# The first low passes of a group one slot on, layer 2's weight pairs in other slots, and the last two pieces on VectorE

## The reference

```python
X = np.fft.rfft(x, axis=1)                       # along the 3008 tokens
y = np.fft.irfft(X * (filt_r + 1j * filt_i), n=x.shape[1], axis=1)
x = y.reshape(6016, 256)
h = x @ w_in                                     # layer 1: 256 -> 2048
g = np.maximum(h, 0) + alpha * np.minimum(h, 0)
x = g @ w_out                                    # 2048 -> 256
h = np.maximum(x @ w_in2, 0)                     # layer 2
out = h * h @ w_out2
```

## Time and profile before

| | |
|---|---|
| median of three runs | 1165.58 us |
| the profiled execution, its own time | 1166.48 us |
| its span, first to last instruction | 1164.7 us |
| TensorE busy | 1130.4 us, 97% |
| VectorE busy | 971.0 us, 83% |
| ScalarE, GpSimd busy | 654.2 and 606.6 us |
| mean granted TensorE clock | 0.991 |

### The profile page before, as it was taken

The page is one execution under the profiler, slowest core; times in us unless marked ns, Lnnn a source line. Parts: engine busy times, 40 slices in busy tenths (PEclk is TensorE's granted clock), DMA queues, the critical chain, the costliest instruction groups (busy, mean ns, idle before and its releaser), DMA issues.

```text
span 1164.7 us, 17117 instructions
## 1 busy us (share of the span) xinstructions
PE 1130.4 (97%) x6867; PEld 984.8 (85%) x6867; DVE 971.0 (83%) x1116; ACT 654.2 (56%) x769; POOL 606.6 (52%) x440
## 2 busy tenths in 40 slices
PE   7879999999999999999999999999999999999997
PEld 2556888888898898898899899998999989889896
DVE  0769788888878988989888988889888888888886
ACT  4746556565655555555555555555555555555553
POOL 0605544555555665566564554555455455555544
PEclk9989999999999999999999999999999999999999
DMA  8973352544203204313135801101101110110100
GB/s 246 280 232 96 95 142 61 122 119 101 57 28 106 87 21 131 106 44 106 50 107 183 283 3 37 36 1 36 37 7 31 36 36 1 36 37 1 37 18 18
DMA packets 64304, 93.45 MB, mean 80 GB/s; under 512 B 5344, under 2 KB 50272, under 8 KB 64224
## 3 DMA queue, kind: packets, MB, share of 16 engines
q1 hardware_dynamic: 64224, 92.35, 27.4%
HBM read 55.90 MB, written 36.44 MB: 79 GB/s over the span
## 4 chain that ended last, share of the span: by engine, by line
PE 75%; DVE 11%; ACT 4%; issue 4%; DMA 4%; POOL 1%; SPq 0%; POOLq 0%; DVEq 0%; ACTq 0%; PEldq 0%
PE bank L875 13%; PE bank L880 13%; PE bank L876 13%; PE bank L905 12%; PE bank L900 10%; PE bank L898 10%; DVE g_lo L746 4%; PE bank L857 3%; ACT g_hi L503 3%; DVE ct L735 1%; DVE ct L731 1%; DMA v_rows<-v_out_b 1%; DVE ct L740 1%; PE bank L831 1%; PE bank L825 1%
## 5 line engine op out<-in xcount | busy, mean ns | idle before, releaser
L491 POOL TENSOR_TENSOR g_raw<-g_raw 128x250 f32<-128x250 f32 (+1 forms) x192 | 277.1, 1443 | 474.2 <-DVE g_raw L769 474.2
L746 DVE TENSOR_TENSOR g_lo<-g_raw,g_hi 128x1750 fp32r<-128x1750 f32 (+1 forms) x192 | 419.9, 2187 | 38.9 <-ACT g_hi L503 37.6
L594 ACT ACTIVATE g_raw<-bank 128x500 f32<-128x500 f32 (+1 forms) x384 | 226.8, 591 | 378.3 <-PE bank L880 377.1
L503 ACT ACTIVATE g_hi<-g_raw 128x1750 fp32r<-128x1750 f32 (+1 forms) x192 | 320.4, 1669 | 37.8 <-POOL g_raw L494 36.1
L898 PE MATMUL bank<-g_hi,w_hi 128*128 128x250 f32 (+1 forms) x1344 | 321.2, 279 | 1.2 <-ACT g_hi L503 1.2
L900 PE MATMUL bank<-g_hi,w_lo 128*128 128x250 f32 (+1 forms) x1344 | 321.5, 279 | 0.0
L875 PE MATMUL bank<-in_hi,w_hi 128*128 128x500 f32 (+1 forms) x768 | 308.2, 401 | 4.9 <-DVE g_raw L762 4.8
L876 PE MATMUL bank<-in_hi,w_lo 128*128 128x500 f32 (+1 forms) x768 | 298.9, 389 | 0.0
L494 POOL TENSOR_TENSOR g_raw<-g_raw 128x250 f32<-128x250 f32 (+1 forms) x192 | 262.8, 1369 | 15.0
L898 PEld LDWEIGHTS bank<-g_hi,w_hi 128*128 128x128 f32 x1344 | 253.9, 189 | 8.9 <-ACT g_hi L503 1.4
L900 PEld LDWEIGHTS bank<-g_hi,w_lo 128*128 128x128 f32 x1344 | 254.0, 189 | 7.4
(11 more groups left out here) (55 smaller groups left out, 529.1 us busy)
## 6 DMA issues: line engine op xcount, KB each, us to landing
filt_b<-filt SPq DMA_DIRECT2D x36, 256.0 KB, 4.7
vc<-v_rows SPq DMA_DIRECT2D x24, 288.0 KB, 5.0
t_raw_b<-t_rows SPq DMA_DIRECT2D x24, 256.0 KB, 4.5
v_rows<-v_out_b SPq DMA_DIRECT2D x24, 256.0 KB, 3.3
w_rows<-s_hi SPq DMA_DIRECT2D x8, 704.0 KB, 3.8
w_rows<-s_lo SPq DMA_DIRECT2D x8, 704.0 KB, 3.2
w_hi<-w_rows SPq DMA_DIRECT2D x8, 704.0 KB, 4.2
w_lo<-w_rows SPq DMA_DIRECT2D x8, 704.0 KB, 5.7
```

The lines of the kernel that those rows point to most:

```text
L491: pool.tensor_tensor(g_raw[:, r, T2, 0:h], g_raw[:, r, B22, 0:h], g_raw[:, r, T1N, 0:h], ALU.add).then_inc(t2_ready, 1)
L503: return act.activation(dst, src, ACT.Copy)
L594: act.activation(g_raw[:, r, 2 * j:2 * j + 2, 0:h], h_ps[j][:, 0:2 * h].rearrange("p (j d) -> p j d", j=2), ACT.Relu, scale=-1.0 if n < SL ...
L746: dve.tensor_tensor(g_lo[:, q, B11:T4 + 1, 0:h], g_raw[:, q, B11:T4 + 1, 0:h], g_hi[:, q, :, 0:h], ALU.subtract).then_inc(g_lo_ready, 1)
```

## The change

Three things are changed.

1. For n = 8g, g from 1 on, down(n) is cut in two. Its high passes stay in slot n + 2. Its low passes go into slot n + 3, between the two up passes.
2. W2_SLOT, the slots of the eight weight pairs, becomes 37, 43, 50, 58, 66, 74, 82, 90 instead of 40, 46, ... 82. The last store now falls behind layer 1's last slot, so the stores and loads leave the condition on layer 1, and reading back waits for the store of its own pair alone.
3. In the very last slot, VectorE makes the two pieces of L491 and L494, ahead of the g_lo of slot 190.

```diff
-W2_SLOT = [40 + 6 * q for q in range(FP)]
+W2_SLOT = [37, 43, 50, 58, 66, 74, 82, 90]
...
-                    sp.wait_ge(s_stored, 32 * FP)
+                    sp.wait_ge(s_stored, 32 * (q + 1))
...
+                if n == 2 * SLOTS_1 - 1:
+
+                    break
                 pool.wait_ge(t13_ready, n + 1)
                 pool.tensor_tensor(g_raw[:, r, T2, 0:h], g_raw[:, r, B22, 0:h], g_raw[:, r, T1N, 0:h],
...
-            act.wait_ge(t4_ready, 2 * SLOTS_1)
+            act.wait_ge(t4_last, 1)
...
+                if n == 2 * SLOTS_1 - 1:
+                    dve.wait_ge(t13_ready, n + 1)
+                    dve.tensor_tensor(g_raw[:, r, T2, 0:h], g_raw[:, r, B22, 0:h], g_raw[:, r, T1N, 0:h],
+                                      ALU.add).then_inc(t2_last, 1)
+                    dve.wait_ge(t2_last, 1)
+                    dve.tensor_tensor(g_raw[:, r, T4, 0:h], g_raw[:, r, B21, 0:h], g_raw[:, r, T2, 0:h],
+                                      ALU.subtract).then_inc(t4_last, 1)
...
                 for j in range(2):
+                    if j == 1 and late_low(n - LAG - 1):
+                        down_low(n - LAG - 1)
                     if n > 0:
                         pe.wait_ge(g_ready, 2 * n + j - 1)
...
+            def late_low(n):
+                return n > 0 and n % FP == 0
+
+            def down_high(n):
...
+            def down_low(n):
+                g, p = divmod(n, FP)
+                q, h = n % RING, HALF[g % GROUPS]
+                last = p == FP - 1
                 pe.wait_ge(g_lo_ready, n + 1)
...
                 if n >= LAG:
-                    down(n - LAG)
+                    down_high(n - LAG)
+                    if not late_low(n - LAG):
+                        down_low(n - LAG)
```

More of the change, by code:

```diff
@@ L234, in spectral_mix_two_ffn @@
         t13_ready, t2_ready, t4_ready = sem("t13_ready"), sem("t2_ready"), sem("t4_ready")
+        t2_last, t4_last = sem("t2_last"), sem("t4_last")
         g_hi_ready, g_lo_ready = sem("g_hi_ready"), sem("g_lo_ready")
@@ L404, in _ @@
                         load_vc(g + 1)
[L405 to L423, removed]
+                for q in range(FP):
+                    if W2_SLOT[q] + 6 == n:
+                        cols = slice(q * W_T * P, (q + 1) * W_T * P)
+                        sp.wait_ge(s_hi_ready, q + 1)
+                        sp.dma_start(w2_rows[0][:, cols], s_hi[:, :, :].rearrange("p t d -> p (t d)").bitcast(F32)
+                                     ).then_inc(s_stored, 16)
+                        sp.wait_ge(s_lo_ready, len(W2_LOW) * (q + 1))
+                        sp.dma_start(w2_rows[1][:, cols], s_lo[:, :, :].rearrange("p t d -> p (t d)").bitcast(F32)
+                                     ).then_inc(s_stored, 16)
@@ new lines, in _ @@
+                for q in range(FP):
+                    if W2_SLOT[q] == n:
+                        if q > 0:
+                            sp.wait_ge(s_stored, 32 * q)
+                        else:
+                            for s in f1.v_stored:
+                                sp.wait_ge(s, 16 * (B_UNITS // f1.deep + 1))
+                        sp.dma_start(s_raw[:, 0:W_RAW, :].rearrange("p t d -> p (t d)"),
+                                     w2[:, q * W_RAW * P:(q + 1) * W_RAW * P]).then_inc(s_loaded, 16)
@@ L882, in up @@
                     mm.then_inc(h_done, 1)
-            def down(n):
+            def late_low(n):
+                return n > 0 and n % FP == 0
+            def down_high(n):
                 g, p = divmod(n, FP)
                 q, h = n % RING, HALF[g % GROUPS]
-                first, last = p == 0, p == FP - 1
+                first = p == 0
                 pe.wait_ge(g_hi_ready, n + 1)
@@ L941, in _ @@
             for n in range(2 * SLOTS_1 - LAG, 2 * SLOTS_1):
-                down(n)
+                down_high(n)
+                down_low(n)
 def _split(m):
```

## The result

The changed kernel takes 1170.47 us, the median of six runs (1168.78 to 1173.14), the one before 1165.34 (1162.84 to 1166.76). The ratio is 1.0049, 95% interval 1.0033 to 1.0066: slower by 5.7 us (3.8 to 7.7), where the medians alone give 5.1. The forecast was +3.7 and 1169.3.

What follows compares the result with a forecast made beforehand. TensorE, busy 1130.4 of 1164.7 us, was taken as the bound, so only its waits or spared work count. Terms 7.1 - 1.1 + 0.3 - 1.1 - 1.5 = +3.7 on the median 1165.58 gave 1169.3 us, range 1165.4 to 1172.2.

Steps and rivals of the forecast that it cites:

- layer 2 starts, groups 12 to 23: First down slot of twelve groups: TensorE's up pass waits for VectorE's late piece, 6.12 instead of 5.53 us each; +7.1.
- groups 2 to 4: Group starts with two transforms: these fill the time until the piece is done, winning 0.36 each; -1.1.
- groups 5 to 11: Group starts near weight pairs: all become 6.16 us, against 6.40, 6.52, 5.74 and 5.53 before; together +0.3.
- fourth pair's load: SyncE's queue: the store now stands two slots ahead of the load, so VectorE's 1.08 us idle time goes; -1.1.
- the end: Last slot: VectorE makes the last two pieces instead of GpSimd, last low passes start at 1155.8 instead of 1157.26; -1.5.
- The layer 2 stall: Group 13: the piece is done at 708.02, TensorE goes on at 708.08; the start takes 0.59 us longer.
- The sums' slots: Groups 5 to 11: moved weight sums shorten four long starts, moved low passes put nearly the same stall back; +0.3.
- third rival: GpSimd's low parts hit starts of groups 5 to 12: +8 at 1.0 each, 1177, likelier 1172; chance 0.10.
- it evens out: Whole kernel: restart costs nothing, or end and load bring their upper bounds; no change, about 1166.8 us; chance 0.12.
- the wait does not come: First piece of slot 8g+2 done when high passes end, no group start stalls; -15.3, 1150.3 us; chance 0.08.

Runs made afterwards that it cites:

- late_only: The kernel before with the moved low passes alone, old weight-pair slots and old end; 1178.76 us, ratio 1.0116 to the kernel before.
- w2_only: The kernel before with the new weight-pair slots alone, low passes and end as before; 1162.92 us, ratio 0.9979 to the kernel before.
- no_low_two: The changed kernel without GpSimd's low parts for the first and last weight pair, high parts stored twice; 1169.83 us, ratio 1.0033 to the kernel before.
- piece_first: The changed kernel with VectorE making the first piece of slot 8g+2 ahead of the g_lo; 1151.08 us, ratio 0.9879 to the kernel before.

## Why the prediction was right

The sign and the mechanism held. The size came out somewhat short: +3.7 forecast, +5.0 by the traces and +5.7 by the ratio, whose interval begins at 3.8. By the forecast's terms, from the traces (the sum holds 0.1 that lies in no term):

| term | forecast | measured |
|---|---|---|
| layer 2 starts, groups 12 to 23 | +7.1 | +7.6 (eleven at 0.57 to 0.61, group 12 at 1.11) |
| groups 2 to 4 | -1.1 | -1.0 |
| groups 5 to 11 | +0.3 | +1.1 (group 5 alone +0.53, -0.24 forecast) |
| fourth pair's load | -1.1 | -1.17 |
| the end | -1.5 | -1.56 |
| sum | +3.7 | +5.0 |

- *The layer 2 stall.* The earlier trace rows gave 2.48 from the first high matmul to the up matmul; the trace has 2.49. What carried the forecast was one row that cost nothing at the time: the pieces that began at 707.36 and that nobody waited for.
- *The sums' slots.* The forecast said that new slots would take away what makes starts long and the moved passes would put it back. late_only and w2_only show the two halves: 7.2 and 5.5 at groups 6 and 9, and 6.15 together.
- *The parts and the whole.* Alone the parts come to +13.5, -2.4 and -0.7 (+11.7, -2.95 and -1.0 by the traces), +7.8 by the traces in sum where the whole is +5.0. Most of these 2.7 us is no interplay of the parts: 1.6 is the drop of the clock in late_only's group 8, which no other trace has in the stretches compared, and 0.9 the stall in slot 94, which w2_only has and the changed kernel has not. In the changed kernel VectorE begins the two operations on the input at 639.90, before that low part (641.13) and not behind it. Where neither is at work, the moved passes cost the same with the old slots as with the new: 0.63, 0.68 and 0.64 at groups 7, 10 and 11 between before and late_only, 0.64, 0.68 and 0.64 between w2_only and the change. From slot 8's first high matmul to slot 184's it is +8.9 with the new slots (974.53 against 965.59) and +11.1 with the old, 9.5 of them without the drop of the clock.
- *The term that was mis-sized* is the third rival, GpSimd's low parts at group starts. The forecast had them at nothing, the rival at 1.0 for each of eight starts. They came at two: +0.77 at group 5, all of which no_low_two takes away, and +0.48 at group 12, of which it takes 0.27. What the other 0.2 at group 12 is stays open. Groups 6 to 11 were not touched: 6.15 to 6.19 with low parts just before. So these two starts make up 1.25 of the 1.3 by which the forecast was short by the trace, and 1.04 of that is shown to be the low parts'.
- The rival had the place right and the path wrong. The forecast spoke of VectorE operations held up by a low part. At group 5 it is GpSimd's own next operations that come late, then one of them meets VectorE's g_lo: 2.35, where the same operation in no_low_two, begun before the g_lo, takes 0.73.
- The Trainium skill ("SBUF — State Buffer", section "SBUF: two separate sides") says that where a VectorE operation with two inputs in SBUF meets a GpSimd operation that reads SBUF, the one that starts first gets the shared port pair for its whole instruction. The trace agrees with that order: L498 began 0.80 after the g_lo and ended 0.59 after it. The g_lo itself began 0.01 behind GpSimd's other operation (L495, at 340.15) and took 2.56, where it takes 1.97 in slot 106. A count of instructions that can meet is no price, though; in the changed kernel, of eight starts with low parts near them two paid.
- *Rival "it evens out"* fails: the restart costs its 0.1 also when the up pass comes first (from the up matmul at 705.29 to the next first high matmul it is 3.63, where the same matmuls without a pause take 2.71 + 0.81 = 3.52). *Rival "the wait does not come"* is what piece_first makes true: it had 1150.3, piece_first measured 1151.1. That they are so near is partly luck. By the trace piece_first gains 11.1 and not the rival's 15.3: layer 2's starts stay at 5.14 to 5.27 and group 5's at 5.59, and 2.6 goes in stretches that the rival did not name.
- The 0.7 between +5.0 of the traces and +5.7 of the ratio lies within its interval.

## What to carry to other kernels

When work is moved away from in front of a wait, look at what it was covering: here the next thing to be late stood one row further down in VectorE's timeline, with no idle time anywhere to mark it. Two engines' orders often have to be changed together; on top of the new slots each of two edits cost 9 to 12 us alone, and both together gave 6. And a group of small operations without a deadline (the weight pairs) belongs in the slots where the engine has no backlog from a group start.

## What the runs showed of the hardware

A pause of TensorE in the middle of full work was once followed by a drop of its clock. In late_only, group 8, VectorE made the four sums first and then the piece, and TensorE stood idle for 1.78 us until 489.69. VectorE, then TensorE of late_only (L908 a high pass, L880 an up pass, L918 the low passes):

```profile
487.86 0.28 DVE L672 SCALAR_TENSOR_TENSOR s_raw<-s_raw 128x128 f32<-128x128 f32 x1
...
488.91 1.37 DVE L763 SCALAR_TENSOR_TENSOR g_raw<-g_raw,rest_sb,bank 128x500 f32<-128x500 f32 x2
```

```profile
487.64 0.28 PE L908 MATMUL bank<-g_hi,w_lo 128*128 128x250 f32 x1
489.69 0.49 PE L880 MATMUL bank<-in_hi,w_hi 128*128 128x500 f32 x1 [1.78 <-DVE g_raw L763]
...
491.30 1.69 PE L918 MATMUL bank<-g_lo,w_hi 128*128 128x250 f32 x7
492.79 0.63 PE L880 MATMUL bank<-in_hi,w_hi 128*128 128x500 f32 x1
```

The same kernel's table by stretches (us, busy times, then PEclk, the granted clock, DMA share and GB/s):

```profile
489.70:492.00 2.30, 2.30 (x10) 2.02 (x11) 2.27 (x3) 0.71 (x1) 0.92 (x1) 0.78 1.17 205
492.00:494.00 2.00, 2.00 (x8) 1.79 (x8) 1.18 (x2) 0.59 (x1) 1.92 (x2) 0.50 0.74 305
494.00:496.00 2.00, 2.00 (x14) 1.81 (x13) 0.72 (x2) 0.90 (x2) 1.53 (x2) 0.90 0.00 0
```

From 491.30 the seven low passes take 1.49 up to the next matmul, where 0.81 is usual. Read in steps of half a microsecond, the granted clock is 1.00 until 491, 1.3 us after TensorE had started again, and 0.50 from 491 to 494, the lower of TensorE's two levels (1.2 GHz); from 494.5 on it is full. With 8.77 this start is 1.6 longer than its like in groups 5, 6 and 9.

The length of the pause does not decide it alone. The same trace has three more pauses as long, before the same matmul of groups 5, 6 and 9 (1.79, 1.72 and 1.75 us), and over the 8 us behind each of them the granted clock stays at 1.00. The one of group 5:

```profile
352.28 0.49 PE L880 MATMUL bank<-in_hi,w_hi 128*128 128x500 f32 x1 [1.79 <-DVE g_raw L763]
```

Nor did the 1.53 at group 5 of the changed kernel [its rows above] bring such a drop. That the pause of group 8 caused the drop is therefore not shown, and what sets group 8 apart is open. Other executions of late_only may have had more of them: the profiled one has the highest mean granted clock of the six, 0.991, and the shortest time, 1177.10; the others have 0.985 to 0.988 and 1178.01 to 1181.05. That could explain the time of +13.5 beside a trace of +11.7, but the kernel before spreads from 0.988 to 0.994 too, and those executions have no trace, so it is not shown.
